# Top-k attention and two MoE layers: penalty ahead of the exponent, scores on both array halves, V stationary, x made transposed

## The reference

```python
scores = (q @ k^T) / 8                        # 2 batches, 8 heads, 576 tokens, head size 64
kth    = 32nd largest of each row             # rows of 576 scores
scores = where(scores >= kth, scores, -1e9)
attn   = softmax(scores); x = attn @ v        # x: 1152 tokens x 512
x2     = silu(x @ w_in) @ w_out               # hidden size 2048
P      = exp(x2 @ w_gate), 8 rounds of row and column scaling
out    = sum over 8 experts e of P[:, e] * (relu(x2 @ w1[e]) @ w2[e])   # hidden size 1024
```

## Time and profile before

| | us |
|---|---|
| median of three runs | 1368.88 |
| span of the profiled execution | 1366.2 |
| busy PE / DVE / ACT / POOL in it | 1350.0 / 733.3 / 490.3 / 351.1 |
| longest wait of PE | 5.2, for the first inputs |

### The profile page before, as it was taken

One profiled execution on the slowest core, in us unless ns is written; L12 is line 12 of the kernel. 1 busy time (PEld: TensorE's weight loads), 2 busy tenths in 40 slices (PEclk: granted clock), 3 DMA queues, 4 the chain that ended last, 5 costly groups with the idle time before them and its releaser, 6 DMA issues.

```text
span 1366.2 us, 21083 instructions
## 1 busy us (share of the span) xinstructions
PE 1350.0 (99%) x8021; PEld 1197.5 (88%) x8021; DVE 733.3 (54%) x1561; ACT 490.3 (36%) x1040; POOL 351.1 (26%) x305
## 2 busy tenths in 40 slices
PE   8999999999999999999999999999999999999999
PEld 6887888788878889989989989989989988998997
DVE  6999989998999975652222222222222222222222
ACT  3446766766675645402112202202211211211210
POOL 0004434534553543212112202202202211211200
PEclk9999999999999999999999999999999999999999
DMA  2033223222231223211011001001101101101001
GB/s 55 23 95 110 89 66 114 84 84 86 90 119 54 93 94 124 93 63 62 19 44 62 31 31 61 31 30 61 61 0 61 61 0 61 61 17 45 0 0 69
DMA packets 59745, 82.16 MB, mean 60 GB/s; under 512 B 17568, under 2 KB 25760, under 8 KB 59680
## 3 DMA queue, kind: packets, MB, share of 16 engines
q1 hardware_dynamic: 59680, 81.30, 18.5%
HBM read 78.92 MB, written 2.36 MB: 59 GB/s over the span
## 4 chain that ended last, share of the span: by engine, by line
PE 94%; DVE 3%; DMA 1%; ACT 1%; issue 1%; POOL 0%; SPq 0%; ACTq 0%
PE banks L322 24%; PE banks L323 24%; PE banks L324 23%; PE banks L377 6%; PE banks L353 5%; PE banks L450 4%; PE banks L361 3%; PE banks L371 2%; PE banks L333 2%; PE banks L336 1%; PE banks L349 1%; DVE rest L747 1%; DVE stats L736 1%; DVE probs L757 1%; PE banks L391 0%
## 5 line engine op out<-in xcount | busy, mean ns | idle before, releaser
L970 POOL TENSOR_TENSOR wu_lo<-wu_raw,wu_hi 128x512 fp32r<-128x512 f32 x116 | 148.7, 1307 | 725.1 <-ACT wu_hi L639 718.3
L696 ACT ACTIVATE h_hi<-banks 128x384 fp32r<-128x384 f32 x192 | 94.5, 492 | 617.4 <-PE banks L324 617.4
L871 DVE SCALAR_TENSOR_TENSOR h_lo<-banks,h_hi 128x384 fp32r<-128x384 f32 x192 | 106.8, 557 | 281.3 <-ACT h_hi L696 281.3
L322 PE MATMUL banks<-x_lo,wu_hi 128*128 128x384 f32 x768 | 257.3, 335 | 0.0
L324 PE MATMUL banks<-x_hi,wu_hi 128*128 128x384 f32 x768 | 256.8, 334 | 0.0
L323 PE MATMUL banks<-x_hi,wu_lo 128*128 128x384 f32 x768 | 256.7, 334 | 0.0
L913 DVE SCALAR_TENSOR_TENSOR y_acc<-banks,plan_e,y_acc 128x512 f32<-128x512 f32 x135 | 101.4, 751 | 265.1 <-PE banks L324 265.1
L323 PE MATMUL banks<-wd_hi,h_lo 128*128 128x512 f32 x576 | 226.8, 394 | 0.0
L322 PE MATMUL banks<-wd_lo,h_hi 128*128 128x512 f32 x576 | 226.0, 392 | 0.0
L324 PE MATMUL banks<-wd_hi,h_hi 128*128 128x512 f32 x576 | 223.7, 388 | 0.0
L970 POOL TENSOR_TENSOR wd_lo<-wd_raw,wd_hi 128x512 fp32r<-128x512 f32 x112 | 144.7, 1313 | 93.7 <-ACT wd_hi L639 93.7
(11 more groups left out here) (100 smaller groups left out, 1979.6 us busy)
## 6 DMA issues: line engine op xcount, KB each, us to landing
wu_raw<-in_moe_w_in_dram SPq DMA_DIRECT2D x16, 1024.0 KB, 5.3
wd_raw<-in_moe_w_out_dram SPq DMA_DIRECT2D x16, 1024.0 KB, 5.4
wu_raw<-in_moe_w_dram SPq DMA_DIRECT2D x16, 1024.0 KB, 5.0
wd_raw<-in_moe_w_dram SPq DMA_DIRECT2D x16, 1024.0 KB, 5.2
k_nat<-in_k_dram SPq DMA_DIRECT2D x32, 128.0 KB, 2.0
v_nat<-in_v_dram SPq DMA_DIRECT2D x32, 128.0 KB, 2.3
q_nat<-in_q_dram SPq DMA_DIRECT2D x32, 72.0 KB, 2.2
out_dram<-y_acc SPq DMA_DIRECT2D x9, 256.0 KB, 2.0
```

Of the source, the lines that this page charges most:

```text
L322: pe.matmul(to, a_hi, b_lo, start=first, stop=False)
L696: act.activation(h_hi[:, f, CH * c:CH * (c + 1)], ps_up[:, at % UBANKS, 0:CH], ACT.Relu).then_inc(h_hi_done, 1)
L871: dve.scalar_tensor_tensor(h_lo[:, f, toks], ps_up[:, at % UBANKS, 0:CH], 0.0, h_hi[:, f, toks].bitcast(F32), ALU.max, ALU.subtract).then_ ...
L970: pool.tensor_tensor(w_lo[stream][:, slot, piece, :], raw[stream][:, piece, :], w_hi[stream][:, slot, piece, :].bitcast(F32), ALU.subtract ...
```

## The change

Six things are changed, all in the attention stage.

1. The mask goes. DVE multiplies the largest and the 32nd largest score by two factors (`least_kept`). ACT then forms relu(2^94 * (kth - score)) over the tile (`penalise`), POOL subtracts it from the scores (`lower_scores`), and only then ACT takes the exponent, with the sum (`exp_scores`).
2. Keys lie in two halves of 288 on partitions 0 to 63 and 64 to 127, and queries are loaded twice beside each other, so the two score products of a tile use different rows of the array.
3. V is the stationary operand. Two heads share a "unit" (five units of two heads or a rest tile in half a quarter), their outputs on columns 0 to 63 and 64 to 127. x comes out transposed, the transposes of the output go, and ACT's scaling becomes a spread of the inverse sums by PE (`spread_sums`) and a product on DVE (`scale_output`).
4. Keys and values are loaded in every other quarter; q has one buffer, whose load waits until the head before is transposed.
5. Tiles are ordered by pairs of heads, slices and weight pieces come one step later, and the high and low parts of x are made by ACT and POOL from `xt_f32`.
6. SP's list of loads is in another order.

```diff
-    rows = [(GROUP * g + j, r) for j in range(GROUP) for r in range(2)]
-    TILES += rows[:-1] + [(g, REST_TILE)] + rows[-1:]
+    for pair in (2 * g, 2 * g + 1):
+        TILES += [(2 * pair + j, r) for r in range(2) for j in range(2)]
+    TILES += [(g, REST_TILE)]
...
+                if z == 0:
+                    for c in range(2):
+                        sp.dma_start(k_nat[:, h % 2, :, c, :], k_h[b, h, c]).then_inc(arrived, 16)
+                    need(sp, o_done, units_of_group(qr - 1, h // GROUP))
...
+                need(sp, heads_t, hh)
+                for c in range(2):
+                    sp.dma_start(q_nat[:, :, c, :], q_h[b, h, z]).then_inc(arrived, 16)
...
             for qr in range(QUARTERS + 1):
-                head(qr, 3)
-                down(qr - 1, 1)
                 up(qr - 1, 2)
                 head(qr, 4)
+                down(qr - 1, 1)
+                head(qr, 5)
                 down(qr - 1, 2)
-                head(qr, 5)
                 up(qr - 1, 3)
...
                 down(qr - 1, 4)
+                head(qr + 1, 2)
                 up(qr - 1, 5)
-                head(qr + 1, 2)
+                head(qr + 1, 3)
...
+                    for c in range(2):
+                        last = pe.matmul(ps_s[:, c, 0:KHALF], q_half(hh, c, slice(P * r, P * (r + 1))), k_half(h, c),
+                                         start=True, stop=True)
...
-                        last = pe.matmul(ps_t[:, 1, O:O + D], pT[0:keys_in(c), c, :], v_nat[0:keys_in(c), h, c, :],
-                                         start=(c == 0), stop=(c == KC - 1))
+                        for j in range(2):
+                            last = pe.matmul(ps_t[D * j:D * (j + 1), 1, XO:XO + P],
+                                             v_nat[0:keys_in(c), h - 1 + j, c, :],
+                                             pT[0:keys_in(c), (tile - 1 + j) % 2, c, :],
+                                             start=(c == 0), stop=(c == KC - 1))
...
+            def spread_sums(tile):
...
+                pe.wait_ge(rinv_ready, tile + 1)
...
+                    for j in range(2):
+                        last = pe.matmul(ps_kq[D * j:D * (j + 1), 1, RO:RO + P],
+                                         stats[:, (tile - 1 + j) % 2, 35:36].to_broadcast([P, D]), ident[:, :],
+                                         start=True, stop=True)
+                last.then_inc(r_done, 1)
...
+                silu_slice(slice_at(step - 1, 0))
                 if step < NT:
                     keep_clock(ps_m[:, 1, 0:P], 4)
...
+                if 0 <= step - 3 < ALL:
+                    spread_sums(step - 3)
                 if step + 1 < ALL:
                     scores_of(step + 1)
...
+                if old:
+                    transpose_probs(step - 2)
+                transpose_head(head_at(step + 2), units_by(step - 3))
...
+                silu_slice(slice_at(step - 1, 1))
...
+                if old:
+                    weigh_values(step - 2)
...
+            def penalise(tile):
...
+                act.wait_ge(kth_ready, tile + 1)
+                need(act, pT_done, tile - 1)
+                act.activation(probs[:, tile % 2, 0:S], scores[:, tile % 3, :], ACT.Relu,
+                               bias=stats[:, tile % 2, 33:34], scale=-PENALTY).then_inc(penned, 1)
...
+                act.wait_ge(lowered, tile + 1)
+                act.activation(probs[:, tile % 2, 0:S], probs[:, tile % 2, 0:S], ACT.Exp,
+                               bias=stats[:, tile % 2, 32:33], scale=D ** -0.5,
+                               accum_out=stats[:, tile % 2, 34:35]).then_inc(exp_done, 1)
...
+                    exp_scores(step - 2)
+                g_high(slice_at(step - 2, 0))
+                if 0 <= step - 3 < ALL:
+                    copy_output(step - 3)
+                take_slice(slice_at(step - 1, 0))
                 if step + 1 < ALL:
                     copy_scores(step + 1)
...
                 if 0 <= step - 2 < ALL:
-                    copy_output(step - 2)
-                if step % NT < 2 and NT <= step < ALL + NT:
-                    split_output(step // NT - 1, 2 * (step % NT))
-                split_pieces(pieces_at(step, 0))
-                take_slice(slice_at(step, 1))
-                g_high(slice_at(step, 0))
-                split_pieces(pieces_at(step, 1))
...
+                    copy_pT(step - 2)
+                copy_kq(head_at(step + 2))
+                g_high(slice_at(step - 2, 1))
+                if 0 <= step - 1 < ALL:
+                    penalise(step - 1)
+                split_pieces(pieces_at(step - 1, 0))
+                split_pieces(pieces_at(step - 1, 1))
+                take_slice(slice_at(step - 1, 1))
...
+            def least_kept(tile):
...
+                dve.tensor_tensor(st[:, 32:34], st[:, 0:TOPK:TOPK - 1], factors[:, :], ALU.mult).then_inc(kth_ready, 1)
...
-                dve.scalar_tensor_tensor(probs[:, tile % 2, 0:S], scores[:, tile % 3, :], st[:, TOPK - 1:TOPK],
-                                         probs[:, tile % 2, 0:S], ALU.is_ge, ALU.mult,
-                                         accum_out=st[:, 33:34]).then_inc(summed_by(tile)[0], 1)
...
+            def scale_output(tile):
...
+                dve.wait_ge(o_copied, unit + 1)
+                dve.wait_ge(r_done, unit + 1)
...
+                    dve.tensor_tensor(x, x, ps_kq[:, 1, RO:RO + P], ALU.mult).then_inc(x_scaled, 1)
...
+            def lower_scores(tile):
+                pool.wait_ge(penned, tile + 1)
+                pool.tensor_tensor(probs[:, tile % 2, 0:S], scores[:, tile % 3, :], probs[:, tile % 2, 0:S],
+                                   ALU.subtract).then_inc(lowered, 1)
...
             for step in STEPS:
-                g_low(slice_at(step - 1, 1))
-                if step <= ALL:
-                    split_pieces(pieces_at(step, 0))
-                g_low(slice_at(step, 0))
-                if step <= ALL:
-                    split_pieces(pieces_at(step, 1))
...
+                if 0 <= step - 2 < ALL:
+                    lower_scores(step - 2)
+                g_low(slice_at(step - 2, 0))
+                if step - 1 <= ALL:
+                    split_pieces(pieces_at(step - 1, 0))
+                g_low(slice_at(step - 2, 1))
+                if step - 1 <= ALL:
+                    split_pieces(pieces_at(step - 1, 1))
+                if step % NT == 15 and step < ALL:
+                    output_lows(step // NT, 0)
+                if step % NT == 2 and NT <= step < ALL + NT:
+                    output_lows(step // NT - 1, 2)
```

More of the change, by code:

```diff
@@ L39 @@
 REST = QT - 2 * P
-HEAD_LOADS = 5
 GROUP = P // REST
@@ L122, in slices_done, with rest_tile, unit_ending, unit_of @@
     return 2 * KD * (n // 2) + 4 * (d // 2) + 2 * (n % 2) + d % 2 + 1
+def rest_tile(qr, g):
+    return NT * qr + GROUP_TILES * (g + 1) - 1
+def unit_ending(tile):
+    k = tile % NT % GROUP_TILES
+    if k % 2 == 0 and k < GROUP_TILES - 1:
+        return None
+    return unit_of(tile)
+def unit_of(tile):
+    return GROUP_UNITS * (tile // GROUP_TILES) + tile % GROUP_TILES // 2
+def units_by(tile):
+    return unit_of(tile) + (unit_ending(tile) is not None) if tile >= 0 else 0
+def heads_by(tile):
+    return H * (tile // NT) + sum(r == 0 for _, r in TILES[0:tile % NT + 1]) if tile < ALL else H * QUARTERS
+def units_of_group(qr, g):
+    return GROUP_UNITS * (2 * qr + g + 1)
+def head_at(tile):
+    if tile < ALL and TILES[tile % NT][1] == 0:
+        return H * (tile // NT) + TILES[tile % NT][0]
+    return None
+def loads_of(hh):
+    return sum(6 if i // H % 2 == 0 else 2 for i in range(hh % 2, hh + 1, 2))
 def need(eng, sem, count):
@@ L324, in three_passes, with transpose_head @@
                 return pe.matmul(to, a_hi, b_hi, start=False, stop=last)
[L326 to L333, removed]
+            def transpose_head(hh, spread):
+                if hh is None:
+                    return
+                h = hh % H
+                pe.wait_ge(qkv_in[h % 2], 16 * loads_of(hh))
+                need(pe, kq_ready, hh)
+                need(pe, x_scaled, spread)
+                if hh // H % 2 == 0:
+                    for w in range(QC):
+                        pe.transpose(ps_kq[:, 0, KROWS * w:KROWS * (w + 1)], k_nat[:, h % 2, w, :, :].rearrange("p c d -> p (c d)"),
+                                     ident[0:KROWS, 0:KROWS])
                 for c in range(QC):
-                    at = KTAIL + QROWS * c
-                    last = pe.transpose(ps_kq[0:D, 1, at:at + QROWS], q_nat[0:QROWS, h % 2, c, :],
+                    last = pe.transpose(ps_kq[:, 1, QROWS * c:QROWS * (c + 1)],
+                                        q_nat[:, c, :, :].rearrange("p c d -> p (c d)"),
                                         ident[0:QROWS, 0:QROWS])
@@ L341, in scores_of @@
                 h, r = TILES[tile % NT]
+                hh = H * (tile // NT) + h
                 if r == 0:
```

(17 more changed lines are left out.)

309 lines of the change are left out of this document (150 added, 159 removed).

## The result

The changed kernel takes 1519.57 us, the median of four runs (1517.69 to 1523.39), against 1368.67 us for the kernel before on the same chip (the median of four runs of it there). The ratio is 1.1105, with a 95% interval from 1.1088 to 1.1121. The profiled execution has a span of 1515.7 us, 149.5 us over that of before. The forecast of 1494 us was 26 us short, and the time lies in its range.

The account below looks back on a forecast made before the run. PE and DVE bound the kernel before; a closed ACT-POOL loop would set the changed steps. Quarters +7.2 (with start), +36.2, +37.7, +33.7 and end +10.3 give +125.1 on 1366.2, 1491.3; median 2.7 above: 1494 us, range 1425 to 1535.

Parts of the forecast that it names:

- the first quarter: First quarter of the attention stage: 110.7 us against 105.8, or +7.2 with the start.
- the start: Start of the attention stage: head 1's queries wait for head 0's transpose, and PE for them, 2.3 us.
- long quarters: Quarters two to four of the attention stage: 160.9, 163.6 and 152.2 us, so +36.2, +37.7 and +33.7.
- the end: From the last scores copy to the last quarter's first slice: 32.4 us against 22.1, so +10.3.
- The second MoE layer: The layer from about 560 us on: same work, so its time stays.
- The loop through ACT and POOL: Attention steps: penalty, pieces, subtraction, exponent form a closed loop; 9.4, 7.9 or 10.5 us with pieces, 5.8 without.
- Loads: SP's late loads for steps 3 and 17: six ACT waits of about 4.5 us, one of about 1.
- The unknown costs: Attention stage: exponent's sum and Relu penalty each 0 to 0.2 us extra, taken as 0; POOL's subtraction 1.43 us.
- The fast rival: Attention stage: chain hidden, PE and DVE bound, some 105 us a quarter, 1324 us in all; chance 0.14.
- PE's slower level: Attention steps with pieces: waits halve PE's pace, 29 us more a quarter, 87 in all, 1581 us; chance 0.10.

Follow-up runs that it names:

- sub_first: The changed kernel with the subtraction and the step's second g_lo moved ahead of both calls for weight pieces in POOL's list: 1372.76 us.
- sub_mid: The changed kernel with the subtraction placed between POOL's two calls for weight pieces: 1446.99 us.
- sp_order: The changed kernel with the loads for steps 3 and 17 moved ahead of a head's loads in SP's list: 1502.72 us.
- best: The changed kernel with sub_first's and sp_order's edits (old order behind last quarter), fourth up unit's pieces from step 13, step-17 load earlier still, 640-byte pad: 1344.05 us.
- fill: The changed kernel with 12 unused identity products on PE ahead of the transposes of probs, in steps where those wait for POOL's pieces: 1521.52 us.

## Why the prediction was right, point by point

The mechanism and its price in a step were right. That the total came within 26 us owes something to errors of opposite sign: 11.7 us too much for the first quarter with the start, against 21.8 too little for the three long quarters, 6.2 for the end, 0.3 for the slices and 7.8 for the second layer.

- *The loop through ACT and POOL.* Right, shown by sub_first and sub_mid. Distances of scores copies in the second quarter: up steps with pieces 9.1 to 9.6 us (forecast 9.4), others with two pieces 7.9 to 8.9 (7.9), with four 10.4 and 10.7 (10.5), without pieces 4.8 to 6.7 (5.8). Apart from these stand the two steps with a load wait (12.9 and 13.9), the one in which x is split (9.5), and the one with the first low parts of x on POOL (10.5).
- *The first quarter.* Wrong by the sum's largest single error: -6.1 and -4.5 with the start, where I had +4.9 and +7.2. Its 15 steps, put at 5.5 us, took 5.1 on average, with 3.3 and 3.4 us at the start: 6.2 us. The last three took 23.4 us where 28.2 were put. That sum held a load wait of 4.5, which falls into the second quarter's window (it ends at 119.30 us). The start cost 1.6 (2.3).
- *The long quarters.* +40.9, +45.5 and +43.0 us against +36.2, +37.7 and +33.7. The fourth has two full load waits (5.4 and 4.7 us), where one and 1 us more were put; this 4.6 is what the first quarter had too much. The step in which x of the finished quarter is split takes 9.5 to 10.4 us (forecast 8.1), and one step without pieces takes 8.5 and 8.3 in the last two quarters (5.8). The rest is spread over many steps. The longest step, behind a load wait and the sums, is 16.5.
- *Loads.* Right in size and number: 4.88 us in the row above, six waits worth 25 us in sp_order. One of them was put in the wrong quarter, as said.
- *The end.* From the last scores copy to the first slice 38.6 us (610.3 to 648.9), 16.5 more than before; forecast +10.3. The 24 gate products in it now all stand at its end and take 6.5 us; in the kernel before, 12 of them ran earlier, from 500.3 us, and 12 right before the slices, in 2.2 us. The first 15 also start 0.32 us apart and not 0.17, so PE's lower level costs some 2 us here.
- *The second MoE layer.* "Has the same work and stays" is a step whose reasoning failed: +7.8 us, from 640 bytes of address. With -4.5, +129.4, +16.5, +0.3 of slices and +7.8 the sum is the 149.5 us measured.
- *The unknown costs.* The exponent's sum adds a READ_ACCUMULATOR of 0.19 us, of which 0.09 before the next start: inside the 0 to 0.2 I allowed. The subtraction takes 1.40 us (1.43).
- *The fast rival.* Wrong for this list, but it is what remains of the change once the subtraction stands first. Its size was too hopeful: 105 us a quarter, where best has 109 to 120 (109 for 17 steps).
- *PE's slower level.* It came (0.79 to 0.83), as the Trainium skill ("TensorE: Matmul & The Clock Gate", "HAM oscillation — how this bites in real kernels") says of waits between bursts, but did not set the time: in fill, at 0.91 to 0.93, 42 of 53 steps were 6.3 us shorter together, and the end lost some 2 us to it; the rival had put 87. PE's slack hides most of it.

## What to carry to other kernels

Before an operation of a critical item goes to an engine that has time to spare, write down what stands ahead of it in that engine's list and who releases that. Idle time that is spent waiting for the very engine that will wait for you is not free time. Where two engines hand work to each other, add up one turn of the loop and compare it with the step; here 9.4 against 5.7 us told the result, and moving the subtraction ahead of the pieces was worth 147 us.

## What the runs showed of the hardware that was not expected

- *Addresses.* Products with 128x512 moving operands started 233 to 234 ns apart in the changed kernel, and 226 to 232 before. Moving h_hi, h_lo and y_acc by 640 or 384 bytes switched the layer between 806.2 and 814.0 to 814.2 us, both ways.
- *A small DVE operation beside POOL.* The product of two elements a partition by two factors takes 0.14 us in all 52 cases in which POOL is idle beside it. In 18 of the 20 others it takes 0.34 to 0.80, here while POOL's subtraction of 1.40 us that began at 173.87 runs:

```profile
174.61 0.68 DVE L837 TENSOR_TENSOR stats<-stats,factors 128x2 f32<-128x2 f32 x1
```

It has two inputs in SBUF. By the Trainium skill ("SBUF — State Buffer", "Who interferes with whom") such an instruction contends with a GpSimd one that reads SBUF, and the row agrees. The chain did not pay for it here: the ten times that the penalty waited for this product, 3.6 us together, it took 0.14 us.
